# The low-weight tail products of a unit's two halves on the two half-height row tiles of the array

## The reference

```python
# conv: out[b, s, h, g] = sum_k w[h, k] * x_pad[b, s + k, h, g], w = softmax(weight)
h = x @ w_in1                                   # 8192 x 192 by 192 x 2048
h2 = h * h
h3 = h2 * h
P = a[0] + a[1] * h + a[2] * h2 + a[3] * h3
Q = 1.0 + np.abs(b[0]) * np.abs(h) + np.abs(b[1]) * h2
x = (P / (Q + 1e-06)) @ w_out1                  # 8192 x 2048 by 2048 x 192
h = x @ w_in2
r = np.maximum(h, 0.0)
out = (s * (r * r) + b2) @ w_out2
```

## Time and profile before

| what | value |
|---|---|
| median of three runs | 1423.11 us (1421.7 to 1423.2) |
| profiled execution, its own time | 1422.24 us |
| its span, first to last instruction | 1420.4 us |
| mean granted TensorE clock | 0.983 of full speed |
| TensorE matmul busy | 1287.8 us, 91% |
| VectorE busy | 1253.6 us, 88% |
| ScalarE busy | 1107.3 us, 78% |
| GpSimd busy | 329.1 us, 23% |

### The profile page before, as it was taken

One profiled execution on the slowest core, in us unless ns is written; L12 is line 12 of the kernel. 1 busy time (PEld: TensorE's weight loads), 2 busy tenths in 40 slices (PEclk: granted clock), 3 DMA queues, 4 the chain that ended last, 5 costly groups with the idle time before them and its releaser, 6 DMA issues.

```text
span 1420.4 us, 17013 instructions
## 1 busy us (share of the span) xinstructions
PE 1287.8 (91%) x6064; PEld 1080.0 (76%) x6064; DVE 1253.6 (88%) x1232; ACT 1107.3 (78%) x1085; POOL 329.1 (23%) x143
## 2 busy tenths in 40 slices
PE   1557799999999999999999999999999999999998
PEld 0445677878878787888878787887878778787888
DVE  5899999899999989899998989999998999999830
ACT  2568678888888888888888888888888888887843
POOL 2044222222222222222222222222222222222210
PEclk9888899999999999999999999999999999999999
DMA  7010000000000000000000000000000000000000
GB/s 181 30 41 0 0 12 0 24 0 23 0 11 11 3 19 0 22 0 13 10 11 11 0 22 0 22 0 11 11 0 22 0 22 0 11 11 0 12 12 12
DMA packets 23567, 20.99 MB, mean 15 GB/s; under 512 B 1530, under 2 KB 23034, under 8 KB 23034
## 3 DMA queue, kind: packets, MB, share of 16 engines
q1 hardware_dynamic: 23264, 20.72, 5.1%
q10 hardware_dynamic: 282, 0.01, 0.0%
HBM read 14.43 MB, written 6.29 MB: 15 GB/s over the span
## 4 chain that ended last, share of the span: by engine, by line
issue 44%; PE 24%; POOL 14%; DVE 12%; ACT 4%; DMA 1%; ACTq 0%; POOLq 0%; DVEq 0%
POOL gl L278 14%; PE o L329 7%; PE h L303 3%; PE h L307 2%; PE h L306 2%; PE h L305 2%; PE h L304 2%; DVE work L628 2%; DVE work L660 2%; ACT work L489 2%; DVE work L662 1%; DVE work L630 1%; PE o L316 1%; DVE conv L542 1%; PE o L317 1%
## 5 line engine op out<-in xcount | busy, mean ns | idle before, releaser
L278 POOL TENSOR_TENSOR gl<-work,gh 128x1024 fp32r<-128x1024 f32 x128 | 308.4, 2409 | 1008.9 <-ACT gh L493 1008.9
L329 PE MATMUL o<-v,work 128*128 128x192 f32 x2048 | 358.6, 328 | 18.7 <-ACT work L508 18.7
L329 PEld LDWEIGHTS o<-v,work 128*128 128x128 f32 x2048 | 335.8, 190 | 43.6 <-ACT work L508 37.1
L303 PE MATMUL h<-x_hi,w_hi 128*128 128x512 f32 x512 | 225.5, 440 | 62.5 <-DVE work L635 28.4
L628 DVE SCALAR_TENSOR_TENSOR work<-work,coef,h 128x1024 f32<-128x1024 f32 x128 | 163.4, 1277 | 69.1 <-ACT work L489 68.4
L493 ACT CAST gh<-work 128x1024 fp32r<-128x1024 f32 x128 | 134.0, 1047 | 97.9 <-DVE work L666 97.2
L307 PE MATMUL h<-x_tail,w_tail_lo 128*128 128x512 f32 x512 | 205.0, 400 | 0.0
L305 PE MATMUL h<-x_hi,w_lo 128*128 128x512 f32 x512 | 204.9, 400 | 0.0
L306 PE MATMUL h<-x_tail,w_tail_hi 128*128 128x512 f32 x512 | 204.7, 400 | 0.0
L487 ACT ACTIVATE work<-h,coef 128x1024 f32<-128x1024 f32 x128 | 153.7, 1200 | 65.4 <-PE h L307 51.6
L304 PE MATMUL h<-x_lo,w_hi 128*128 128x512 f32 x512 | 204.6, 400 | 0.0
(11 more groups left out here) (70 smaller groups left out, 1695.6 us busy)
## 6 DMA issues: line engine op xcount, KB each, us to landing
x_tok<-in_x_dram SPq DMA_DIRECT2D x18, 384.0 KB, 3.2
out_dram<-y_out SPq DMA_DIRECT2D x16, 384.0 KB, 2.5
work<-in_moe_w_in_dram SPq DMA_DIRECT2D x2, 1024.0 KB, 6.5
work<-in_moe_w_in_dram SPq DMA_DIRECT2D x4, 512.0 KB, 8.3
work<-in_moe_w_out_dram SPq DMA_DIRECT2D x1, 1536.0 KB, 16.1
v<-in_moe_w_out_dram SPq DMA_DIRECT2D x1, 1536.0 KB, 19.3
cw<-in_weight_dram ACTq DMA_DIRECT2D x2, 3.3 KB
cw<-in_weight_dram ACTq DMA_DIRECT2D x2, 0.2 KB
```

What stands on the lines that cost most here:

```text
L278: nc.gpsimd.tensor_tensor(gl[:, j % 2, :], r_buf[j % 2], gh[:, j % 2, :].bitcast(F32), ALU.subtract).then_inc(gl_ready, 1)
L303: pe.matmul(h[:, half, :], hi[:, c], x_hi[:, :], start=True, stop=False)
L329: last = pe.matmul(o2[:, c // 2, c % 2, 0:D], g, v2[:, f, :], start=(f == 0 and c % 2 == 0), stop=(f == FT - 1), skip_group_check=True)
```

## The change

`first_product` keeps four matmuls for a half as they are. The fifth, with the low tail weight, is taken out of the loop over the halves and comes behind both: that of the first half uses rows 0:64 of weight and input, that of the second half rows 64:128. Each multiplies the low tail weight by the high tail input only, so the product of the two low parts is no longer computed. Since high input rows stand in only one half of `x_tail`, a new pair of tiles `tail_copy` takes the other: for layer 1 a transfer copies rows 64:128 of `x1_tail` to rows 0:64 of `tail_copy`, for layer 2 rows 0:64 of `x2_tail` to rows 64:128. SyncE issues both for every tile, and TensorE waits for `x1_copied` and `x2_copied` before the first matmul of a tile in the layer. To make room, `work2` loses a part: the ReLU writes into the `g2` buffer, the square is made in place, and `raw_v1` moves into `work1`, with a wait of ScalarE for `v1_lo_ready` ahead of the first unit.

```diff
-        work2 = sb("work2", [P, 3, W])
-        u_relu = work2[:, 0]
-        g2 = [work2[:, 1], work2[:, 2]]
+        work2 = sb("work2", [P, 2, W])
+        g2 = [work2[:, 0], work2[:, 1]]
...
-        raw_v1 = work2[:, 0:3].rearrange("p a b -> p (a b)").rearrange("p (f d) -> p f d", f=FT)
+        raw_v1 = work1[:, 5:8].rearrange("p a b -> p (a b)").rearrange("p (f d) -> p f d", f=FT)
...
+        tail_copy = [sb(f"tail_copy{i}", [P, TOK], F32R) for i in range(2)]
...
+            def copy_x1_tail(t, parity):
+                sp.wait_ge(x1_hi_ready, counted((t + 1) * 2))
+                sp.dma_start(tail_copy[parity][0:TAIL, :].bitcast(F32),
+                             x1_tail[parity][TAIL:P, :].bitcast(F32)).then_inc(x1_copied, 16)
+
+            def copy_x2_tail(t, parity):
+                sp.wait_ge(x2_tail_hi_ready, counted(t + 1))
+                sp.dma_start(tail_copy[parity][TAIL:P, :].bitcast(F32),
+                             x2_tail[parity][0:TAIL, :].bitcast(F32)).then_inc(x2_copied, 16)
+
+            copy_x1_tail(0, 0)
...
+                if tile(t - 1):
+                    copy_x2_tail(t - 1, 1 - parity)
                 if tile(t - 2):
                     sp.wait_ge(y_ready_out, counted((t - 1) * 2))
...
+                if tile(t):
+                    copy_x1_tail(t + 1, 1 - parity)
...
-                    last = pe.matmul(h[:, half, :], tail_lo[:, c], x_tail[:, :], start=False, stop=True)
+                for half, rows in enumerate((slice(0, TAIL), slice(TAIL, P))):
+                    c = slice((2 * k + half) * P, (2 * k + half + 1) * P)
+                    last = pe.matmul(h[:, half, :], tail_lo[rows, c], high_rows[half], start=False, stop=True)
...
+                    pe.wait_ge(x1_copied, counted((t + 1) * 16))
...
+                            pe.wait_ge(x2_copied, counted((t2 + 1) * 16))
...
+            act.wait_ge(v1_lo_ready, 2)
...
-                        nc.scalar.activation(u_relu, h2_flat, ACT.Relu).then_inc(u_ready, 1)
+                        act.wait_ge(out2_done, counted(m - 1))
+                        nc.scalar.activation(g2[buf], h2_flat, ACT.Relu).then_inc(u_ready, 1)
                         act.wait_ge(u_ready, counted(m + 1))
-                        act.wait_ge(out2_done, counted(m - 1))
-                        nc.scalar.activation(g2[buf], u_relu, ACT.Square).then_inc(g2_ready, 1)
+                        nc.scalar.activation(g2[buf], g2[buf], ACT.Square).then_inc(g2_ready, 1)
```

More of the change, by code:

```diff
@@ L164, in conv_rational_relu2_kernel @@
         y_ready_out = sem("y_ready_out")
+        x1_copied, x2_copied = sem("x1_copied"), sem("x2_copied")
         head_rows = []
@@ L248, in phase @@
                     sp.dma_start(rows.rearrange("(c p) d -> p c d", p=P), y_out[:, :, :]).then_inc(y_stored, 16)
+                if tile(t):
+                    copy_x1_tail(t + 1, 1 - parity)
             run(sp, phase)
             sp.wait_ge(y_stored, 16 * TILES)
+            sp.wait_ge(x1_copied, 16 * (TILES + 1))
             sp.wait_ge(x_loaded, 16 * (TILES + 2))
@@ L415, in phase @@
                         first_product(h2, k2, w2_hi, w2_lo, w2_tail_hi, w2_tail_lo,
-                                      x2_hi[x2p], x2_lo[x2p], x2_tail[x2p], h2_ready)
+                                      x2_hi[x2p], x2_lo[x2p], x2_tail[x2p],
+                                      (x2_tail[x2p][0:TAIL, :], tail_copy[x2p][TAIL:P, :]), h2_ready)
                     if not tile(t):
```

5 lines of the change are left out of this document (3 added, 2 removed).

## The result

The changed kernel takes 1436.08 us (median of four runs, 1435.53 to 1437.92); the kernel before took 1422.47 beside it on the same chip. The ratio is 1.0091, 95% interval 1.0079 to 1.0103. It is slower by 13.6 us, and the prediction said 7.8 faster. The profiled execution took 1435.71 with a span of 1433.9, 13.5 longer than before.

A forecast was written before the change was run, and what follows sets the result against it. TensorE and VectorE take turns as bound, TensorE counting only from unit 4 to unit 7. Fourteen tiles at -0.48 (-6.7), end -1.8 and opening +0.7 sum to -7.8: 1415.3 us for the median, range 1408 to 1444.

The forecast's parts named there:

- VectorE's three waits: VectorE idle before line 628 at units 4, 5 and 7 of a tile: 1.29, 0.98 and 2.10 us.
- c: TensorE's cost for each change between full array and half-height form, two in a product; taken 0, bounds 0 to 0.29 us.
- s: What a first product on TensorE gets shorter: 0.15 - 2c, taken as 0.15 us.
- its costlier form: TensorE emptying beyond c about 0.16: loads exposed too, c = 0.29, s = -0.43, 1496 us; chance 0.09.
- The second rival: TensorE empties at each change before and behind the pair: c = 0.16, s = -0.17, 1440.5 us; chance 0.30.
- the end at 2.0: The emptying rival's loss over the twelve first products after layer 1 has finished: 2.0 us.
- Its opening of 0.7: The emptying rival's loss at the program's start, where the first first-product waits for `x1_copied`: 0.7 us.
- The copy for layer 2: TensorE's first layer 2 unit waits for `x2_copied`: issue 0.19, landing 1.9 (1.6 to 2.5), at 737.20 against 737.08 wanted.
- e: How much later TensorE starts the layer 2 product waiting for its copy: 0.12 us, from -0.18 to 0.72.
- The parts at nothing: Later layer 1 copies, output store in SyncE, ReLU's wait for `out2_done`, in-place square: counted at no cost.
- The first copy of layer 1 in the opening: The first first-product waits for `x1_copied`, landing 38.4 to 39.3 against a 38.12 start: +0.7 us.
- the signs named for a wrong forecast: Over 0.3 around the pair, copy wait over 0.4 at unit 4, more busy TensorE, VectorE waits at units 0 to 3.

The follow-up runs named there:

- the first run: The kernel before with only the memory edits (`work2` of two parts, square in place, `raw_v1` in `work1`, wait for `v1_lo_ready`): 1422.1 us, ratio 0.9995.

## Why the prediction was wrong

**What was read rightly.** VectorE's three waits tell where TensorE's time counts, and the change acts at units 5 and 7; units 0 to 3 stayed VectorE's. Not right was which products count: unit 7 has one pair queued ahead of its product and not two, and a product's own pair counts for nothing (above). TensorE's slack in the other units took up the price of the pairs there: sixteen times 0.17 is 2.7 in a tile, of which 0.48 was paid.

**The step that failed is the value of c.** The prediction took c = 0 for a change of form, "because no row shows TensorE paying when the next matmul is of another shape". The row it rested on was one of line 307 and line 329: 512 and 192 columns, the same 128 rows. That is a change of size, not of the rows in use. No row bore on the rows in use, and the value was taken from the end of the range that favoured the change. The runs give 0.10 on the way in and 0.20 with 0.11 for the following load on the way out, 0.41 for both. Against them stands the one matmul of 0.23 that the overlap saves. So one change costs 0.20 on average, inside the prediction's bounds of nothing and 0.29, and s = 0.23 - 0.41 = -0.17 by the unrounded distances.

The other term of s was off too, and to the other side. The prediction put the second half 0.08 behind the first, for its weight load, so that the pair saved 0.15 and not 0.23; the halves start 0.00 to 0.01 apart. The two figures that it took from the matmuls of line 329, 0.154 for a load and 0.13 for a late one, are misread as well: in the trace those matmuls start 0.16 apart, not 0.154, the first of line 303 only 0.03 behind the last of them (737.05 to 737.08), and the next 0.36 behind that. Together the last two steps are 0.39, as one step of 0.16 and one of 0.23 would be, so the 0.13 is no cost there.

By the Trainium skill, page "TensorEngine Tiling (Array Packing)", section Key Properties, changing the tiling mode drains TensorE. The prediction cited that rule against itself and gave it 0.30, and 0.09 to its costlier form. The trace agrees that the change costs time, 0.10 before and 0.20 behind the pair. That TensorE empties altogether it doesn't show: by the modelled lengths the pair starts at 744.46 and the full matmul ahead of it ends at 744.53. The page "TensorE: Matmul & The Clock Gate", Part 3, has matmuls on different row groups run concurrently, and a weight load pulled ahead where its row group doesn't conflict or where it goes to the background weight buffer. The trace agrees with the first, 0.00 to 0.01 between the two halves. With the second it agrees between full matmuls, where the load at 743.90 begins under the matmul of 743.89; the loads at 744.46 and 744.89, across a change of form, are not pulled ahead.

**The second rival was the case.** It gave s = -0.17 at c = 0.16 and 1440.5. Measured s is -0.17, and the time 1436.1. That s came out to the hundredth is luck: 0.15 - 0.32 and 0.23 - 0.41 have no term in common. A tile's sum was too high: it priced unit 4 too, which does not move because a product's own pair doesn't delay that product, it counted two pairs at unit 7, and it let the slack of a tile run out, which it does not (TensorE is busy 79.92 of 82 us). It said 1.05 a tile, and 0.76 was measured; the end at 2.0, measured 1.8. Its opening of 0.7 is taken up below.

**The copy for layer 2.** Landing was taken at 1.9 (1.6 to 2.5) and is 2.2. Issue was taken at 0.19, from a store that waits, and is 0.03 here (740.11 to 740.14), so from the end of the tail's high part to the landing it is 2.23 where 2.09 was taken. In the tile at 740 TensorE's 16 matmuls would end at 739.70 + 2.57 (the distance at 1388.77), 742.27, and the product starts at 742.39: 0.12 late, which is e as taken, but against a TensorE that is itself behind. In the other phase it is 0.42 later still, from the waits queued behind the one for the copy; that is inside e's upper end of 0.72, but not for the reason given there, a late landing. That the two phases differ was not foreseen, and the expectation ahead of the run with full tail matmuls still put it down to a register instruction. Alone the copy and its wait make 0.52 a tile, and the form 0.48; together 0.76, since the form delays TensorE's arrival at the wait.

**The parts at nothing** stayed at nothing: the memory edits by the first run, ReLU's wait, the store in SyncE's queue. The first copy of layer 1 in the opening was taken as 0.7. The 0.6 between the two traces looks like it but is luck: counted from the cast ahead of the copy the product is 1.0 late and VectorE's first unit 1.3, less the 0.75 by which that execution was ahead. The copy landed 2.28 behind its issue there (35.85 to 38.13), and the product started 0.23 after that.

The range, 1408 to 1444, holds 1436.1. The sign was wrong: 0.40 stood for faster and 0.39 for slower, which says that the evidence did not separate them; a rule against the change and no row for it should have made c = 0.16 the forecast. Of the signs named for a wrong forecast two came: more than 0.3 on both sides of the pair (0.33 and 0.43), and more busy time of TensorE.

## What to carry to other kernels

Two half-height matmuls side by side save one matmul of 0.23, but each change between the full and the split array costs about 0.2, so a single pair between full matmuls loses 0.17. By this arithmetic it pays only if two or more pairs stand together for one change in and one out, which no run here tried. When an operation is of a kind that the trace doesn't show, and a rule says that it costs something, take its price from the nearest rows and not as zero. When a wait of one engine bounds a stretch, count which delays are queued ahead of the awaited operation since the engine's last restart: two pairs at unit 5, one at unit 7, none at unit 4 gave each unit's loss to 0.05. When one of several waits ahead of an operation is fulfilled last, look at what stands behind it: three waits that were long fulfilled cost 0.42 in every second tile here.

## What the runs showed of the hardware

- The two half-height matmuls start 0.00 to 0.01 apart, and take 0.49 to 0.50 by the profile's model where a full one takes 0.40. On the same rows the next full matmul comes 0.24 later than behind a pair side by side.
- Full to half is 0.33 to 0.34 between starts, half to full 0.42 to 0.43 and the next 0.34, whether one half or a pair stands between. In the opening of the changed kernel, where full matmuls are 0.43 apart, the steps are 0.56 (41.48 to 42.04) and 0.72 (42.04 to 42.76), 0.13 and 0.29 too many: the bubbles grow less than the matmuls' own distance does, 0.23 to 0.43. The windows give a granted clock of 1.00 there too, so the trace doesn't say why that distance is 0.43.
- A copy of 128 KB from one on-chip tile to another lands 2.2 us after its issue, where 384 KB to and from memory took 2.5 and 3.2. A third of the bytes saved 0.3 against the store.
- TensorE's instructions that only wait start 0.11 apart once their conditions are met (659.36 to 659.68). A wait that sits on a product's weight load lets it start 0.04 after the landing.
